# One take of three sums moved by one step on VectorE, and two small tensors exchanged in SBUF

## The reference

```python
p = domain_probs / (domain_probs.sum(-1, keepdims=True) + 1e-9)
for e in range(4):                       # w1: 512 x 1024, w2: 1024 x 512
    h = np.maximum(x @ w1[e], 0.0)
    out += p[:, e:e + 1] * (h @ w2[e])
h = out @ w_in                           # 512 x 2048
g = h * np.cos(h)
return g @ w_out                         # 2048 x 512
```

## Time and profile before

| | us |
|---|---|
| median of 3 runs | 643.01 |
| lowest and highest | 642.55, 643.29 |
| the profiled execution: its own time | 643.01 |
| the profiled execution: its span | 641.1 |
| PE busy | 630.0 (98% of the span) |
| DVE, POOL, ACT busy | 305.9, 269.5, 258.8 |

### The profile page before, as it was taken

The page is one execution under the profiler, slowest core; times in us unless marked ns, Lnnn a source line. Parts: engine busy times, 40 slices in busy tenths (PEclk is TensorE's granted clock), DMA queues, the critical chain, the costliest instruction groups (busy, mean ns, idle before and its releaser), DMA issues.

```text
span 641.1 us, 10145 instructions
## 1 busy us (share of the span) xinstructions
PE 630.0 (98%) x3656; PEld 564.2 (88%) x3656; DVE 305.9 (48%) x722; ACT 258.8 (40%) x554; POOL 269.5 (42%) x404
## 2 busy tenths in 40 slices
PE   7899999999999999999999999999999999999998
PEld 5687889999999999999999999999999999999996
DVE  6655331215433315433415333426775666756674
ACT  6685412233321133321233321246554467555452
POOL 6683336597730187730187730277100059400000
PEclk9999999999999999999999999999999999999999
DMA  9855200003210011110021120033100012001011
GB/s 277 273 179 143 103 1 1 1 14 119 67 66 1 1 64 67 65 65 0 1 65 66 66 66 1 2 121 109 34 0 1 0 42 92 1 0 49 0 51 50
DMA packets 21896, 37.25 MB, mean 58 GB/s; under 512 B 2784, under 2 KB 14048, under 8 KB 21856
## 3 DMA queue, kind: packets, MB, share of 16 engines
q1 hardware_dynamic: 20688, 36.71, 17.6%
q10 hardware_dynamic: 1168, 0.02, 0.1%
HBM read 34.36 MB, written 2.36 MB: 57 GB/s over the span
## 4 chain that ended last, share of the span: by engine, by line
PE 95%; DVE 3%; issue 1%; ACT 1%; POOL 0%; DVEq 0%
PE bank L1151 31%; PE bank L1179 31%; PE bank L1210 15%; PE bank L1196 14%; PE bank L1143 2%; PE bank L1107 1%; PE bank L1127 1%; DVE s_sb L821 1%; PE bank L1293 1%; PE bank L1332 1%; ACT prob L574 0%; DVE acc L970 0%; DVE w_hi L846 0%; DVE p_now L872 0%; ACT x_hi L587 0%
## 5 line engine op out<-in xcount | busy, mean ns | idle before, releaser
L424 POOL TENSOR_TENSOR w_lo<-w_raw,w_hi 128x128 fp32r<-128x128 f32 (+1 forms) x252 | 149.4, 627 | 207.8 <-ACT w_hi L606 205.7
L1151 PE MATMUL bank<-x_hi,w_hi 128*128 128x384 f32 (+1 forms) x384 | 132.1, 344 | 0.2 <-DVE x_lo L850 0.2
L1151 PE MATMUL bank<-x_hi,w_lo 128*128 128x384 f32 (+1 forms) x384 | 129.7, 338 | 0.0
L1151 PE MATMUL bank<-x_lo,w_hi 128*128 128x384 f32 (+1 forms) x384 | 129.0, 336 | 0.0
L1179 PE MATMUL bank<-w_hi,hp_hi 128*128 128x512 f32 x288 | 114.4, 397 | 0.3 <-DVE acc L880 0.3
L1179 PE MATMUL bank<-w_hi,hp_lo 128*128 128x512 f32 x288 | 113.4, 394 | 0.0
L1179 PE MATMUL bank<-w_lo,hp_hi 128*128 128x512 f32 x288 | 112.0, 389 | 0.0
L924 DVE TENSOR_TENSOR h_raw<-bank,h_raw 128x384 f32<-128x384 f32 x84 | 46.8, 557 | 97.4 <-PE bank L1196 97.4
L1151 PEld LDWEIGHTS bank<-x_hi,w_hi 128*128 128x128 f32 x384 | 72.2, 188 | 5.3 <-issue 1.0
L1151 PEld LDWEIGHTS bank<-x_lo,w_hi 128*128 128x128 f32 x384 | 72.2, 188 | 3.0
L630 ACT ACTIVATE hp_hi<-h_raw 128x384 fp32r<-128x384 f32 x48 | 25.2, 526 | 117.7 <-DVE h_raw L924 117.7
(11 more groups left out here) (103 smaller groups left out, 963.5 us busy)
## 6 DMA issues: line engine op xcount, KB each, us to landing
w_raw<-in_weights SPq DMA_DIRECT2D x43, 512.0 KB, 3.6
q_t<-in_q SPq DMA_DIRECT2D x12, 192.0 KB, 4.3
result<-acc SPq DMA_DIRECT2D x9, 256.0 KB, 2.1
w_raw<-in_weights SPq DMA_DIRECT2D x8, 256.0 KB, 6.4
k_t<-in_k SPq DMA_DIRECT2D x8, 224.0 KB, 5.2
v_w<-in_v SPq DMA_DIRECT2D x4, 384.0 KB, 4.9
v_w<-in_v SPq DMA_DIRECT2D x4, 320.0 KB, 6.7
k_t<-in_k SPq DMA_DIRECT2D x4, 192.0 KB, 4.2
```

What stands on the lines that cost most here:

```text
L424: last = nc.gpsimd.tensor_tensor(w_lo[:, f, at:at + part], raw[:, at - begin:at - begin + part], w_hi[:, f, at:at + part], ALU.subtract)
L1151: last = nc.tensor.matmul(ps[:, 0:TOK], w[:, f, chunk(c)], x[:, c, token_cols(t)], start=c == 0 and i == 0, stop=c == DC - 1 and i == 2)
```

## The change

Two things are changed. DVE does `take_last_of_experts` in the step of the cosine block's third chunk (i = 2) in place of the second (i = 1). And half_pi and p_now exchange their places among the tensors.

```diff
-        half_pi = sb("half_pi", [P, 1])
+        p_now = sb("p_now", [P, NTOK, OC])
         hp_hi = sb("hp_hi", [P, HP, TOK], F32R)
         hp_lo = sb("hp_lo", [P, HP, TOK], F32R)
         h_raw = sb("h_raw", [P, HP, TOK])
-        p_now = sb("p_now", [P, NTOK, OC])
+        half_pi = sb("half_pi", [P, 1])
...
             for i in range(LAG):
-                if i == 1:
+                if i < LAG - 1:
+                    times_cosine(i, MIX * FC + i, i > 0)
+                else:
                     times_cosine(i, MIX * FC + i, True, take_last_of_experts)
-                else:
-                    times_cosine(i, MIX * FC + i, i > 0)
```

## The result

| | before, us | changed, us |
|---|---|---|
| median (runs) | 643.13 (4) | 651.88 (4) |
| lowest and highest | 642.55, 643.29 | 650.37, 652.26 |
| span of the profiled execution | 641.1 | 648.2 |
| that execution's own time | 643.01 | 650.12 |

The changed kernel takes 1.0134 times as long, interval 1.0115 to 1.0151: 8.75 us more, where 2.2 were forecast (range 644.3 to 646.3). The direction was right, and the stall that was foretold is there. It is about a quarter of the loss.

The account below looks back on a forecast made before the run. PE, a queue of matmuls, was taken as the bound. A stall of 2.05 plus 0.08 for restart, leaned up to 2.2, and zero for the tensor exchange, on 643.0 gave 645.2 us; range 644.3 to 646.3.

Parts of the forecast that it names:

- Where the bound lies: Whole kernel: PE is busy 98% of the span, a queue of matmuls; time lost at the seam moves the end equally.
- Slack and stall: At the seam before down(0): the take's first addition comes 3.79 us later against 1.74 slack, so PE stands 2.05 us.
- the wait for c_u: DVE at the seam: c_k of chunk 2 stands from 443.1 until about 443.44, with the take queued behind it.
- the bounds of the step: DVE's string from c_k to first addition, 2.52 us: lengths varying with POOL's work give a stall of 1.7 to 2.6.
- the stall does not come: Rival at the seam: the take is ready anyway, for instance by c_u of chunk 2 coming sooner; 643.0 us, chance 0.04.
- What else moves with it: Behind the seam: ACT's hp_hi, the w_hi copy, POOL's low part and SP's load come over a microsecond sooner, gaining nothing.
- The exchange of the two tensors: hp_hi, hp_lo and h_raw begin 32 bytes past a multiple of 64; PE's 1296 hp loads were taken to cost zero.
- under the cover: PE's hp loads: 188 ns plus 24 more makes 212, still hidden under a matmul of 230, so cost zero.
- the same 0.45 ns a column, so there is nothing to win back: hp matmuls 0.23 us apart for 512 columns, up-projection 0.17 for 384: equal per column, so no gain from shifted addresses.
- The upper bound of 31 us: Exchange of tensors: 24 ns more on each of 1296 hp loads, all of it laid bare, 31 us.
- The clock: Rival behind the seam's stall: PE falls to 1.2 GHz for 3.36 us, 1.7 us more, 646.9; chance 0.04.
- the row of an idle time of 1.49 us without a fall: Evidence against the clock's fall: PE idled 1.49 us until 8.21, with granted clock 1.00 from 7 to 10.

Follow-up runs that it names:

- the map: PE alone on made-up data, byte addresses of the kernel before, x and hp each put at 8 places, w kept: 4.127 to 4.227 us a pair, 4.167 as before.
- take alone: The kernel before with only the take moved to the third chunk's step, all tensors where they stood: 646.95 us, ratio 1.0056.

## Why the prediction was wrong

**Where the bound lies: right.** PE is the queue, and what it loses stays lost. Both losses show at the end in full, 3.8 + 4.9 against 8.75.

**Slack and stall: right, a little small.** The slack of 1.74 us against a move of 3.79, the wait for c_u, the place of the gap and its releaser were as foretold. 2.37 us were measured against 2.2 taken: hp_lo took 0.81 and not 0.55, which stood in the bounds of the step (1.7 to 2.6). The Trainium skill, SBUF — State Buffer, section "Who interferes with whom", explains such an hp_lo by POOL holding the shared interface. The trace agrees: POOL's pieces run from 444.22 to 452.04, over this hp_lo at 447.99, and the hp_lo of the chunk before, which starts at 444.13, ahead of them, took 0.55. (The rival "the stall does not come" called PE's starts modelled; it is the ends of matmuls that are.)

**What else moves with it: right.** ACT's hp_hi (446.29) and copy to w_hi (446.71) did come sooner against PE, and nobody gained.

**The exchange of the two tensors: the step that failed.** It was taken at zero "under the cover", and cost 4.9 us. Two things were wrong in it. First, the cover: a load 24 ns longer would be hidden under its matmul; but what grew was no load (188 ns in all profiles) but the distance between matmuls, by 4.3 ns. Lengths of loads do not show this. Secondly, "the same 0.45 ns a column, so there is nothing to win back" was an argument from one place of the map, and from rows in steps of 10 ns, coarser than the effect: twelve in 2.11 us are 0.458 ns a column, nine in 2.06 are 0.447. The map has 2.04 to 2.11 us for the nine, and the kernel before stood near its good end. The upper bound of 31 us did contain the cost, but the range left it out with a chance of 0.04. The Trainium skill's lines of 16 bytes (SBUF — State Buffer, section "Specifications (TRN2)") foretold no change for a shift by 32; the runs show one of 0.76%, with a period of 256 bytes, and decide.

**The clock: right in mechanism, wrong in weight.** The rival named the fall by the stall and priced it at 1.7; the rows at half clock give 1.6. It had 0.04, by the row of an idle time of 1.49 us without a fall. In the runs a gap of 2.2 to 2.4 us was followed by the longer time in four of five (take alone) and in five of nine (changed kernel), one of 1.7 in none of five. One gap without a fall was no ground for so small a chance to a gap half as long again.

The sum with what was measured: 643.1 + 2.4 + 4.9 = 650.4 where the clock holds (650.12 to 650.91 measured), and 652.0 where it falls (651.7 to 653.1; the 653.09 lists a mean clock of 0.995, lower than the rest, so probably two falls).

**Left open.** What in the chip makes 256 bytes the period, and why these distances are good, is not shown; the map is a table, not a mechanism. That it needs no other engine is shown. Nor is it shown what makes the clock fall in one execution and not in the next.

## What to carry to other kernels

On a kernel bound by PE, the addresses of loaded and moving operands against each other are a parameter. Here it was worth 1.4% of the kernel's time (639.7 to 648.5 us by pads alone) and 2.4% of the map's: a declaration moved, or one small tensor put in, changes all that lies behind it. Hold the addresses when you compare two kernels, and map the distances with PE alone (one run gives 64) before tuning them. And when an instruction on whose result PE waits is put behind another in an in-order queue, compare what that other one waits for, and the work up to the result, with the slack; where a gap as long as this one (2.3 to 2.4 us) comes out, add the chance that the clock falls behind it, which is paid by the work that follows.

## What the runs showed of the hardware

- Matmul distance depends on the relative byte places of the loaded and the moving operands, with a period of 256 bytes: nine with 512 columns in 2.04 to 2.11 us, twelve with 384 in 2.08 to 2.12, for 4.127 to 4.227 together. The same figures hold with all other engines at work and with none.
- The recorded length of a weight load (188 ns) does not show it.
- A place matters to neighbours that do not read the tensor: x moved by 32 bytes put the down-projection from 2.06 to 2.07 or 2.08, most of it (6 of 10 ns) in the distance to the first matmul that reads x.
- PE's granted clock can fall to 0.50 behind a gap of 2.4 us in an otherwise full stream, in some executions and not in others, at a cost of 1.6 us where it was seen.
- It falls in some executions in the first 25 us too: from 12 to 16 us at no cost in one profile, around 19 us at 1.3 us in another.
